# Router logits of the last chunk with the expert vectors stationary, turned back by four small transposes, and the ranks taken one step later

## The reference, cut to what matters

```
xn = x / (norm(x) + 1e-06)                  # x: 3072 x 512
en = expert_emb / (norm(expert_emb) + 1e-06) # 8 x 512
logits = xn @ en.T / tau
expert_idx = np.argmax(logits, axis=1)
probs = softmax(logits)
out[mask] = gate_w[mask] * (relu(x[mask] @ w1[e]) @ w2[e])
```

## Time and profile before

| | |
|---|---|
| median of 3 runs | 953.38 us (952.11 to 953.56) |
| the profiled execution's own time | 952.52 us |
| its span, first to last instruction | 950.6 us |
| busy: TensorE matmul, VectorE, ScalarE, GpSimd | 99%, 68%, 32%, 26% |
| granted TensorE clock, mean | 0.998 |
| instructions | 16233 |

### The profile page before, as it was taken

The page is one execution under the profiler, slowest core; times in us unless marked ns, Lnnn a source line. Parts: engine busy times, 40 slices in busy tenths (PEclk is TensorE's granted clock), DMA queues, the critical chain, the costliest instruction groups (busy, mean ns, idle before and its releaser), DMA issues.

```text
span 950.6 us, 16233 instructions
## 1 busy us (share of the span) xinstructions
PE 939.7 (99%) x5702; PEld 799.2 (84%) x5702; DVE 648.2 (68%) x1150; ACT 305.1 (32%) x419; POOL 246.7 (26%) x192
## 2 busy tenths in 40 slices
PE   8999999999999999999999999999999999999996
PEld 7888888888888888888888888899999999888885
DVE  5555579647974698558965887776765557799641
ACT  4222121112111121112111221245555557678541
POOL 4443115331434134422433222520000001100101
PEclk9999999999999999999999999999999999999999
DMA  8431297023001400140002202179866667799611
GB/s 305 163 128 62 79 397 236 1 89 134 0 0 44 177 0 0 41 147 12 1 12 89 111 1 89 46 269 318 333 229 222 230 224 278 294 353 379 236 42 55
DMA packets 32032, 138.44 MB, mean 146 GB/s; under 512 B 5183, under 2 KB 5567, under 8 KB 23248
## 3 DMA queue, kind: packets, MB, share of 16 engines
q1 hardware_dynamic: 24464, 119.20, 34.6%
q0 software_dynamic: 4336, 12.61, 3.4%
q10 hardware_dynamic: 3168, 5.79, 1.9%
HBM read 124.96 MB, written 28.41 MB: 161 GB/s over the span
## 4 chain that ended last, share of the span: by engine, by line
PE 98%; DMA 1%; DVE 0%; SPq 0%; issue 0%; POOL 0%; POOLq 0%; ACT 0%
PE bank L753 28%; PE bank L771 28%; PE bank L906 16%; PE bank L868 10%; PE bank L846 6%; PE bank L648 2%; PE bank L692 2%; PE bank L664 2%; PE bank L738 1%; PE bank L681 1%; PE bank L883 1%; DMA attention<-in_qk 1%; PE bank L717 0%; DVE en_all L999 0%; PE bank L711 0%
## 5 line engine op out<-in xcount | busy, mean ns | idle before, releaser
L753 PE MATMUL bank<-activations_split,weights_split 128*128 128x512 f32 x1152 | 277.9, 391 | 0.0
L771 PE MATMUL bank<-weights_split,activations_split 128*128 128x512 f32 x1152 | 276.3, 389 | 0.0
L771 PEld LDWEIGHTS bank<-weights_split,activations_split 128*128 128x128 f32 x1152 | 216.1, 188 | 45.1 <-POOL activations_split L1797 0.4
L753 PEld LDWEIGHTS bank<-activations_split,weights_split 128*128 128x128 f32 x1152 | 215.1, 188 | 45.8 <-issue 1.1
L1797 POOL TENSOR_TENSOR activations_split<-scratch,activations_split 128x512 fp32r<-128x512 f32 x84 | 117.0, 1392 | 311.1 <-ACT activations_split L1542 303.7
L1542 ACT CAST activations_split<-scratch 128x512 fp32r<-128x512 f32 x96 | 59.8, 623 | 412.3 <-DVE scratch L1042 412.3
L906 PE MATMUL bank<-weights_split,activations_split 128*128 128x512 f32 (+1 forms) x648 | 158.2, 396 | 0.0
L1037 DVE TENSOR_SCALAR scratch<-bank,alpha 128x512 f32<-128x512 f32 x96 | 71.8, 747 | 99.1 <-PE bank L753 98.6
L906 PEld LDWEIGHTS bank<-weights_split,activations_split 128*128 128x128 f32 x648 | 118.6, 188 | 23.2
L1101 DVE SCALAR_TENSOR_TENSOR attention<-rows,en_all 128x512 f32<-128x512 f32 x140 | 135.0, 1005 | 1.0 <-DMA en_all<-en_rows 1.0
L1262 DVE TENSOR_TENSOR weights_split<-attention,weights_split 128x2048 fp32r<-128x2048 f32 (+1 forms) x45 | 102.3, 2288 | 24.9 <-ACT weights_split L1622 24.8
(11 more groups left out here) (243 smaller groups left out, 715.7 us busy)
## 6 DMA issues: line engine op xcount, KB each, us to landing
attention<-in_w_exp SPq DMA_DIRECT2D x48, 1024.0 KB, 4.9
en_all<-in_w_exp SPq DMA_DIRECT2D x16, 1024.0 KB
attention<-in_kv SPq DMA_DIRECT2D x43, 256.0 KB, 4.1
expert_rows<-in_pad_rows SPq DMA_DIRECT2D x8, 1285.0 KB, 24.5
rows<-in_w_mlp SPq DMA_DIRECT2D x14, 512.0 KB, 3.5
attention<-in_qk SPq DMA_DIRECT2D x12, 512.0 KB, 5.6
rows<-expert_rows ACTq DMA_DIRECT2D x22, 257.0 KB, 2.9
scratch<-in_qk SPq DMA_DIRECT2D x10, 512.0 KB, 3.8
```

What stands on the lines that cost most here:

```text
L753: last = mm(H_ps[f % 2][:, :], win(a, kc, f), x[:, kc, :], start=(k == 0), stop=(k == 3 * KC - 1))
L771: last = mm(bank[j][:, :], x[f % 2][:, j * P:(j + 1) * P], wout(a, f), start=(f == 0 and a == 0 and part_ == "hi"), stop=(f == FB - 1 and ...
```

## The change

The logits of the last chunk are made in one go. The expert vectors are kept in an upper and a lower part side by side (`en_two`, 16 columns, fp32r), and so are the turned rows (`last_part`, in a half of the weight buffer that is free then). With the 16 columns stationary, 512 token columns move: 4 matmuls on the upper and 4 on the lower part of the rows, into one bank. ScalarE copies the 16 x 512 result to SBUF, and four transposes bring it to tokens by 16 columns; VectorE adds the two groups of 8. `last_logits` comes after `up_two(0,1)`, `logits_turned` after `up_two(0,2)`. VectorE's list gains the four lower parts, a copy and an add, and its order changes. TensorE waits for the choice (`s_oh`) ahead of `expert_down(0)`, and `router_rank` with the count stands between `expert_down(0)` and `expert_down(1)`.

```
+            def last_logits():
+                pe.wait_ge(s_xt, due(s_xt, B))
                 for kc in range(KC):
+                    if kc == KC - 1:
+                        pe.wait_ge(s_xtl, due(s_xtl, B))
+                        for n in range(KC):
+                            mm(LT_ps[0:2 * E, :], en_two[:, n, :], last_lo[:, n], start=False, stop=False)
+                    last = mm(LT_ps[0:2 * E, :], en_two[:, kc, :], last_hi[:, kc], start=(kc == 0), stop=(kc == KC - 1))
+                last.then_inc(s_LT, 1)
+
+            def logits_turned():
+                pe.wait_ge(s_lt, due(s_lt, 1))
+                for j in range(B):
+                    last = tr(LG_ps[:, j, :], lt_sb[:, j * P:(j + 1) * P], ident[0:2 * E, 0:2 * E])
                 last.then_inc(s_R2, 1)
...
-            up_two(0, 1, between=last_logits)
+            up_two(0, 1)
+            last_logits()
             up_two(0, 2)
-            router_rank(NC - 1)
-            mm(CNT_ps, ones, seen[:, :, B], start=True, stop=True).then_inc(s_cnt, 1)
+            logits_turned()
             up_two(0, 3)
             pe.wait_ge(s_phi, due(s_phi, NCH))
             pe.wait_ge(s_plV, due(s_plV, NCH))
+            pe.wait_ge(s_oh, due(s_oh, NC))
             expert_down(0, 0, None, between=lambda: x_transpose(0, 2))
+            router_rank(NC - 1)
+            mm(CNT_ps, ones, seen[:, :, B], start=True, stop=True).then_inc(s_cnt, 1)
             expert_down(1, 1, None, between=lambda: x_transpose(0, 3))
...
-                    dve.wait_ge(s_R2, due(s_R2, 4))
-                link(ve.tensor_tensor(L, logits, bc(inv, E), ALU.mult))
+                    dve.wait_ge(s_R2, due(s_R2, 1))
+                    ve.tensor_copy(L2, logits[:, :, 0:E]).then_inc(s_lsum, 1)
+                    dve.wait_ge(s_lsum, due(s_lsum, 1))
+                    ve.tensor_tensor(L2, L2, logits[:, :, E:2 * E], ALU.add).then_inc(s_lsum, 1)
+                    dve.wait_ge(s_lsum, due(s_lsum, 2))
+                link(ve.tensor_tensor(L, L2, bc(inv, E), ALU.mult))
...
-            ve.tensor_copy(enT, EMB_ps)
+            ve.tensor_copy(en_hi, EMB_ps).then_inc(s_en2, 1)
+            dve.wait_ge(s_en2, due(s_en2, 1))
+            ve.tensor_tensor(en_lo, EMB_ps, en_hi.bitcast(f32), ALU.subtract)
             ve.reciprocal(tau_sb[:, :], TAU_ps).then_inc(s_ent, 1)
...
             rows_out(NC - 1)
             link, n = chain(s_tc, 13)
+            h_two_low(0, 0)
+            for j in range(B):
+                dve.wait_ge(s_xt, due(s_xt, j + 1))
+                ve.tensor_tensor(last_part(1, j), last_ps(j)[:, :], last_part(0, j).bitcast(f32), ALU.subtract).then_inc(s_xtl, 1)
             choose_pairs()
+            h_two_low(0, 1)
             for j in range(B):
...
             router_norm(NC - 1)
-            h_two_low(0, 0)
-            router_choose(NC - 1, LG_ps)
-            h_two_low(0, 1)
-            router_gate(NC - 1)
-            router_place(NC - 1)
             h_two_low(0, 2)
             h_two_low(0, 3)
+            router_choose(NC - 1, LG_ps)
+            router_gate(NC - 1)
             split_expert(1, (0,))
             x_lo_part(2, 2)
+            router_place(NC - 1)
             split_expert(1, (1,))
+            x_lo_part(3, 3)
...
             h_two_high(0, 1)
-            exps(NC - 1)
+            act.wait_ge(s_LT, due(s_LT, 1))
+            se.copy(lt_sb, LT_ps[0:2 * E, :]).then_inc(s_lt, 1)
             h_two_high(0, 2)
             h_two_high(0, 3)
+            exps(NC - 1)
```

More of the change, by code:

```diff
@@ L222, in build @@
     tau_in, tau_sb = sb("tau_in", 1, f32), sb("tau", 1, f32)
-    enT = sb("enT", KC * E, f32)[:, :].rearrange("p (k e) -> p k e", k=KC)
+    en_two = sb("en_two", KC * 2 * E, f32r)[:, :].rearrange("p (k e) -> p k e", k=KC)
+    en_hi, en_lo = en_two[:, :, 0:E], en_two[:, :, E:2 * E]
     emb_ss, emb_nrm, emb_inv, emb_half = (sb(n, 1, f32) for n in ("emb_ss", "emb_nrm", "emb_inv", "emb_half"))
@@ L298, in Y_of @@
         return Y_first[hp] if isinstance(c, int) and c == 0 else Y_ps[hp % 2]
-    LG_ps = bank[7][:, 0:B * E].rearrange("p (b e) -> p b e", b=B)
+    LT_ps, lt_sb = bank[7], EN[0:2 * E, 0:TB]
+    LG_ps = bank[6][:, 0:B * 2 * E].rearrange("p (b e) -> p b e", b=B)
     RK_ps = bank[6][:, 0:B * E].rearrange("p (b e) -> p b e", b=B)
@@ L331, in build @@
     s_emb_ld, s_en_st, s_en_all, s_en_last = sem("emb_ld"), sem("en_st"), sem("en_all"), sem("en_last")
+    s_LT, s_lt, s_xtl, s_lsum, s_en2 = sem("LT"), sem("lt"), sem("xtl"), sem("lsum"), sem("en2")
     s_star, s_tail, s_fill = sem("star"), sem("tail"), sem("fill")
@@ L387, in last_ps, with last_part @@
         return bank[j]
-    def last_xT(j):
-        return Y[:, j * TB:(j + 1) * TB]
+    def last_part(a, j):
+        return W[:, HALF + (a * B + j) * DM:HALF + (a * B + j + 1) * DM]
+    last_hi, last_lo = (W[:, HALF + a * B * DM:HALF + (a + 1) * B * DM].rearrange("p (j k c) -> p k j c", j=B, k=KC)
+                        for a in range(2))
     def bc(ap, n):
@@ L712, in last_transpose @@
                 last.then_inc(s_R1, 1)
-            def last_logits(j):
-                pe.wait_ge(s_xt, due(s_xt, j + 1))
+            def last_logits():
+                pe.wait_ge(s_xt, due(s_xt, B))
                 for kc in range(KC):
-                    last = mm(LG_ps[:, j, :], last_xT(j)[:, kc * P:(kc + 1) * P], enT[:, kc, :],
-                              start=(kc == 0), stop=(kc == KC - 1))
+                    if kc == KC - 1:
[8 more added lines that the diff above has]
+                    last = tr(LG_ps[:, j, :], lt_sb[:, j * P:(j + 1) * P], ident[0:2 * E, 0:2 * E])
                 last.then_inc(s_R2, 1)
@@ L850, in up, with up_two @@
                 last.then_inc(s_M1, 1)
-            def up_two(i, g, between=None):
+            def up_two(i, g):
                 slot = i % 2 * HALF
@@ L871, in up_two @@
                             k += 1
-                        if between is not None and kc % 2 and (j, kc) != (1, KC - 1):
-                            between(2 * j + kc // 2)
                 last.then_inc(s_M1, 1)
-                if between is not None:
-                    between(3)
             def h_transpose(t):
@@ L1353, in _ @@
             link(ve.tensor_tensor(early[:, 1:E], t_off[o, 1:E], t_off[o, 0:E - 1], ALU.subtract))
-            x_lo_part(3, 3)
             h_two_low(1, 0)
@@ L1660, in last_copy @@
                 act.wait_ge(s_gl, due(s_gl, FB * NC))
-                se.copy(last_xT(j), last_ps(j)[:, :]).then_inc(s_xt, 1)
+                se.copy(last_part(0, j), last_ps(j)[:, :]).then_inc(s_xt, 1)
             x_hi_part(0, 0)
```

## The result

963.89 us median of 4 runs (963.81 to 965.70) against 952.89 for the kernel before, ratio 1.011 (95% interval 1.009 to 1.013): 11 us slower. The sign and the two new waits were forecast; what these set off was priced at nothing: 958.0 was said, with 961.6 as the upper end. The profiled execution has a span of 961.7 us and a mean granted clock of 0.995.

The account below looks back on a forecast made before the run. TensorE, 98% of the chain, was taken as the bound. Waits of 3.3 + 1.5, together 4.9 us with the 1.2 saving inside, on 952.52 gave 957.4, put at 958.0 towards the runs' median; range 955.8 to 961.6.

Parts of the forecast that it names:

- VectorE's list: VectorE's work from 618.7 to the end of `router_choose`, which releases `expert_down(0)`: 17.0 us, ending at 635.7.
- the two new waits: TensorE waits for the choice ahead of `expert_down(0)` and for the slot numbers ahead of `expert_down(1)`: 3.3 + 1.5 us more.
- The standstill ahead of `expert_down(0)`: TensorE, ready at 630.65, stands still for `s_oh` until 635.8: 5.1 us.
- Ranks and slots between the two `expert_down`: Ranks, `router_place` and handovers ahead of `expert_down(1)` add 1.5 us, bounds 0.6 and 3.
- Eight matmuls: The new logits on TensorE, 512 columns each at 0.23 us: 1.84 us together.
- four transposes: Turning the logits back on TensorE at 0.10 us each: 0.40 us, bounds 0.2 and 0.8.
- The preparation of the expert vectors: One more subtraction ahead of the attention, covered by an 8x512 product: 0, or 0.22 us without the cover.
- Rival (a): TensorE's clock falls through the standstill ahead of `expert_down(0)`: 2 us more, 959.9; chance 0.27.
- rival (b): SyncE's late queue delivers pair 2's weights 2.9 us late: 960.3; chance 0.15, alone or with the low clock.
- The queue's term: SyncE's queue behind the slots falls back 3 us against TensorE, within a slack of 4.6: 0, bounds 0 and 2.9.
- Rival (c): `s_oh` comes by 630.65, ranks hidden, only the 1.2 us saving stays: 951.3; chance 0.04 wholly, 0.05 by half.
- Rival (d): The new logit products run at twice 0.23 us; TensorE is ready at 632.5, total unchanged; no chance given.

Follow-up runs that it names:

- kept_busy: The changed kernel with 18 additional matmuls that nobody reads, placed ahead of the wait for the choice: 961.08 us, ratio 1.007.
- best: The changed kernel with `choose_pairs` first, ranks inside `expert_down(0)`, `router_place` behind `router_gate`, `router_choose` ahead of `h_two_low(0,3)`: 957.87 us, ratio 1.004.
- all_three: The changed kernel with `choose_pairs` first, ranks and count in the middle of `expert_down(0)`, `router_place` right behind `router_gate`: 958.31 us, ratio 1.004.
- ranks_early: The changed kernel with ranks and count right behind the choice wait, ahead of `expert_down(0)`, and `router_place` right behind `router_gate`: 960.20 us, ratio 1.005.
- after_again: The changed kernel run once more, unchanged: 965.23 us, ratio 1.012.
- wait_middle: The changed kernel with the wait for the choice moved from ahead of `expert_down(0)` to its middle: 959.75 us, ratio 1.006.
- before: The kernel without the change: 952.89 us median.
- after: The changed kernel itself, against the kernel without the change: 963.89 us median, ratio 1.011.
- choose_first: The changed kernel with `choose_pairs` back in VectorE's gap, ahead of `h_two_low(0,0)`: 961.08 us, ratio 1.007.

## Why the prediction was right and wrong

- **The bound, the sign and the two waits** were right: TensorE has nothing to fall back on, and its two new waits cost what was worked out. The standstill ahead of `expert_down(0)`: 5.1 said, 5.02 measured. VectorE's list: 17.0 said, 16.9 (619.82 to 636.68). Start of `expert_down(0)`, counted from the first quarter: 3.35 later said, 3.36 measured. Ranks and slots between the two `expert_down`: 1.55 said, 1.49 measured. Eight matmuls: 1.84 said, 1.85 (623.61 to 625.46); four transposes: 0.40 said, 0.35. The preparation of the expert vectors: 0, and the attention behind it starts 0.11 later, a lead that stood there already ahead of the preparation. With these terms alone the sum is 4.9, as forecast.
- **The step that failed is that the clock and the queue were priced at nothing in the sum and set aside as rivals, each priced by itself.** Rival (a) put 2 us on the low clock, and 1.94 came (kept_busy shows 1.7 of it to be the clock); rival (b) put up to 2.9 on the queue, and 2.30 came. Both follow from the late choice: the clock from TensorE's standing still for it, the queue's wait from the slots behind it. The second does not need the first, since best has no standstill ahead of the slots and waits 3.6 us for the weights. Neither takes anything from the other, and both came. 957.4 + 1.9 + 2.3 is 961.7 against the profiled execution's own 963.81, so these two are 4.2 of the 6.4 us that the sum lacked. The forecast gave the queue, alone or with the clock, a chance of 0.15; its upper end of 961.6 covers the two together and nothing more.
- **The queue's term** was mis-sized in two places. The entry that waits for the scatters came 13.5 us behind the slots (15.1 before), not the 10.7 that "falls back by 8" comes to (15.1 less 12.4, plus 8): of the 7.6 us by which the slots fell back against TensorE, 6.0 reached the weights (issued 13.9 later, TensorE 7.9), not 3. And the block issued behind the padding took 9.2 us to land (672.29 to 681.5), and 9.8, 10.0 and 10.1 in all_three, ranks_early and best, where 8.3 was reckoned (658.42 to 666.7). Its landing in the kernel before is in no view. If it took 9.2 to 10.1 there, it was there between 667.6 and 668.5, and the slack was 2.8 to 3.7 rather than 4.6; best's wait gives 3.0. I had read the end of the traffic, and guessed the share of the last block from it.
- **The clock** was called "on the edge" because it fell 4.6 us after the last matmul at the kernel's end. It fell 1.9 us into the standstill here, 3.2 us into the same one in after_again, and in wait_middle after a standstill of 2.1. One row of one fall is no threshold. The Trainium skill, "TensorE: Matmul & The Clock Gate", section "Why this matters for your kernels", warned of long idle gaps between bursts; kept_busy agrees with it (3.02 against 4.71 for twelve matmuls), and the falls behind 2 us show that the gap needn't be long.
- **Slips in the recorded sums.** The end of `choose_pairs` moves by 6.7 us by the layout's own numbers (621.8 less 615.06), not 6.9. The queue's 8 does not follow from its rows: 635.38 and 5 us to landing are 640.4, 5.3 before 645.74, and 12.4 less 5.3 is 7.1; the fall-back would have been 2.2 and still within the slack. Rival (a) on the sum of 957.4 is 959.4, not 959.9. None of them moves the forecast.
- **The remaining 2 us** of the profiled pair, 1.1 ahead of the stage and 0.9 behind it, were no step of the forecast. after_again has 0.3 and 0.3 in these places and more in the stage, with the same sum. That part of them belongs to the change is not excluded; their cause stays open.
- **Rival (c)**, VectorE keeping up, had a floor that I did not see: `h_two_low(0,3)` ahead of the choice makes the wait at least 3.5 us. **Rival (d)** did not happen.

## What to carry to other kernels

When a result is moved behind others in one engine's list and the bounding engine waits for it, write out the whole list ahead of it, as here (17 us against 12), and look for an item that itself waits for the bounding engine: that sets a floor. Then price what else it sets off, the clock behind the standstill and everything that hangs on the late result in a DMA queue, and add these up instead of choosing among them. The 1.2 us of matmul time that the new logits save are in every profile of them. It took four changes of order and two moved queue entries until a whole stage was shorter than before's (75.04 against 76.07, one execution each), and the medians still don't show a gain.

## What the runs showed that was not expected

- The low clock came with standstills of 5.0, 3.6, 3.6, 3.2, 2.1 and 1.96 us and did not come with others of 2.04, 1.87, 1.67 and 0.8. Near two microseconds both happen. From the first quarter of pair 2 to the middle of `expert_down(4)` before takes 14.26 us, after 16.56 and kept_busy 18.01: the same wait of 2.0 cost 2.3 in one kernel and 3.8 in another. The fall came between 1.9 us (after) and 5.3 us (ranks_early) after TensorE had stopped.
- It can begin after work has resumed: in wait_middle TensorE started again at 636.2, and the clock fell around 637.5; so it was in choose_first (634.5 and 635.4), ranks_early (635.2 and 635.4) and kept_busy (683.2 and 684.7). What it costs depends on where it lies: 1.9 us where three of its seven microseconds fell into the standstill (after), 3.3 where all of them lay over work (ranks_early).
- Two executions of the changed kernel differ in places that no edit touches: the first quarter starts at 616.12 and 615.30, and the broadcast of the expert vectors takes 12.2 and 10.1 us to land. So single profiles compare within a stage and not across the span, and even the stage moved by 1.3 us (85.15 and 86.48).
